# Mixer kernel, three stages on one core: x in falling rows, first sums in one bank, V split where it is read

## The reference

```
w = softmax(weight)                                   # 8 heads x 7 taps
out[b,s,h,:] = sum_k w[h,k] * x[b, s-6+k, h, :]        # stage 1: causal convolution along s
x = out
u = x + (U,V low rank along s): h = (x^T @ U @ V)^T    # stage 2
x = u + relu(u @ w_ch1) @ w_ch2
mixed = real(fft(fft(x, axis=s), axis=d))              # stage 3
u = x + mixed; un = (u - mean) / sqrt(var + 1e-6)
out = u + relu(un @ w_ch1') @ w_ch2'
```

## Time and profile before

| | |
|---|---|
| median of three runs | 1252.08 us |
| the profiled execution's own time | 1252.0 us |
| its span | 1250.2 us |
| mean granted TensorE clock | 0.994 |
| PE busy | 1218.4 us (97%) |
| DVE busy | 823.3 us (66%) |
| ACT busy | 645.3 us (52%) |
| POOL busy | 424.6 us (34%) |
| first `up_slot` of block 0 begins | 42.79 us |

### The profile page before, as it was taken

How to read it: one execution, slowest core, us unless ns; L and a number is a source line. 1 busy time by engine, 2 the same in 40 slices (tenths; PEclk the granted TensorE clock), 3 DMA queues, 4 the chain that set the end, 5 groups by cost and what they waited for, 6 DMA issues and landing times.

```text
span 1250.2 us, 23671 instructions
## 1 busy us (share of the span) xinstructions
PE 1218.4 (97%) x8448; PEld 1193.5 (95%) x8448; DVE 823.3 (66%) x2196; ACT 645.3 (52%) x1603; POOL 424.6 (34%) x542
## 2 busy tenths in 40 slices
PE   6799999999999999999999999999999999999998
PEld 5799999999999999999999999999999999999998
DVE  5555576787766577655557777765666877766654
ACT  5355555444566555445555555544445555554553
POOL 0122352244334245333333244421212344533331
PEclk9799999999999999999999999999999999999999
DMA  8867553244556633224434322222323232232220
GB/s 285 263 207 228 181 161 96 78 151 136 160 161 221 210 112 100 75 69 136 135 96 138 115 92 87 92 69 81 96 87 106 86 101 92 92 94 86 87 68 29
DMA packets 87965, 154.86 MB, mean 124 GB/s; under 512 B 11480, under 2 KB 46915, under 8 KB 87804
## 3 DMA queue, kind: packets, MB, share of 16 engines
q1 hardware_dynamic: 80232, 134.35, 34.3%
q0 software_dynamic: 7616, 18.99, 4.8%
HBM read 94.98 MB, written 63.32 MB: 127 GB/s over the span
## 4 chain that ended last, share of the span: by engine, by line
PE 93%; DVE 2%; DMA 2%; issue 1%; POOL 1%; ACT 1%; SPq 0%; POOLq 0%; ACTq 0%
PE bank L804 20%; PE bank L805 9%; PE bank L785 8%; PE bank L792 7%; PE bank L789 7%; PE bank L793 7%; PE bank L786 7%; PE bank L838 4%; PE bank L808 4%; PE bank L886 3%; PE bank L854 2%; PE bank L909 2%; PE bank L856 2%; PE bank L855 2%; PE bank L807 2%; PE bank L870 1%
## 5 line engine op out<-in xcount | busy, mean ns | idle before, releaser
L981 ACT ACTIVATE ht<-bank 128x384 fp32r<-128x384 f32 x528 | 259.0, 490 | 504.3 <-PE bank L793 502.1
L1165 DVE SCALAR_TENSOR_TENSOR ht<-bank,ht 128x384 fp32r<-128x384 f32 x528 | 293.8, 556 | 338.1 <-ACT ht L981 336.8
L804 PE MATMUL bank<-w,ht 128*128 128x384 f32 x1320 | 418.0, 366 | 0.6 <-DVE ub L1173 0.3
L805 PE MATMUL bank<-w,ht 128*128 128x192 f32 x1320 | 330.8, 251 | 0.0
L1409 POOL TENSOR_TENSOR ub<-ub,tmp 128x576 f32<-128x576 f32 x88 | 125.8, 1430 | 463.9 <-DVE ub L1173 313.9
L804 PEld LDWEIGHTS bank<-w,ht 128*128 128x128 f32 x1320 | 248.5, 188 | 3.8 <-issue 3.1
L805 PEld LDWEIGHTS bank<-w,ht 128*128 128x128 f32 x1320 | 252.0, 191 | 0.0
L785 PE MATMUL bank<-uth,w1h 128*128 128x384 f32 x528 | 188.9, 358 | 0.1
L789 PE MATMUL bank<-utl,w1h 128*128 128x384 f32 x528 | 178.9, 339 | 0.3 <-DVE utl L1190 0.2
L792 PE MATMUL bank<-uts,w1s 128*128 128x384 f32 x528 | 178.6, 338 | 0.3
L786 PE MATMUL bank<-uth,w1l 128*128 128x384 f32 x528 | 178.4, 338 | 0.0
(11 more groups left out here) (116 smaller groups left out, 2220.5 us busy)
## 6 DMA issues: line engine op xcount, KB each, us to landing
f1t<-f_copy SPq DMA_DIRECT2D x44, 396.0 KB, 3.3
ub<-x_two SPq DMA_DIRECT2D x44, 288.0 KB, 3.0
mix<-mixed SPq DMA_DIRECT2D x44, 288.0 KB, 3.3
out<-ub SPq DMA_DIRECT2D x44, 288.0 KB
xin<-in_x SPq DMA_DIRECT2D x12, 864.0 KB, 7.2
x_conv<-xin SPq DMA_DIRECT2D x12, 756.0 KB
vch<-v_split SPq DMA_DIRECT2D x44, 192.0 KB, 2.8
mixed<-rowk SPq DMA_DIRECT2D x88, 74.2 KB
```

The lines of the kernel that those rows point to most:

```text
L804: e.matmul(dn[t][:, 0:2 * D], hh, w2[ph][:, m, :], start=(m == 0), stop=False)
L805: mm = e.matmul(dn[t][:, 0:D], hl, w2[ph][:, m, 0:D], start=False, stop=False)
L981: e.activation(hth[q % 4], up[q % 3][:, 0:TOK], ACT.Relu).then_inc(act_h, 1)
L1165: e.scalar_tensor_tensor(htl[q % 4], up[q % 3][:, 0:TOK], 0.0, hth[q % 4].bitcast(F32), ALU.max, ALU.subtract).then_inc(dve_l, 1)
```

## The change

It has three parts, and some moves that go with them.

1. **Falling rows.** The host lays x out so that a tile's rows fall along the partitions. The band then needs diagonals of the other slant, which the DMA from `taps` gives directly: it writes `band`, and `steep`, DVE's copy and the semaphore `band_set` are gone. The convolved rows come out in the same order as before.
2. **First sums in one bank.** For batch 0 the four pieces of x^T U accumulate in one PSUM bank, from the first matmul of piece 0 to the last of piece 3. DVE's four additions to `tacc` and the three that follow become three on 32x192 elements (`first_sum_t`), at the end. Whoever reuses a buffer of a piece waits for a new semaphore, `pe_t0`.
3. **V's first six tiles.** The portions are now tiles 0 to 5, 6 to 14, 15 to 23 and 24 to 32. Portion 0 is made directly in the two `vch` buffers, and `load_v(0)` and `load_v(1)` are gone. It is still written to DRAM (the other batches read it from there), in block 0, slot 0. It is made after all four pieces, no longer in the third. Portion 1 is made in slots 1 and 2 of block 0, and `store_v(1)` moves to slot 3. `load_v(2)` reads tiles 6 to 8, which now belong to portion 1, and so it waits for both stores.

```
-V_PARTS = [(0, 9), (9, 17), (17, 25), (25, N2)]
+V_PARTS = [(0, 2 * TB), (2 * TB, 15), (15, 24), (24, N2)]
...
-    return x[:, first[None, :] + np.arange(N1)[:, None]]
+    return x[:, first[None, :] + np.arange(N1)[::-1, None]]
...
-        vpart = [ht[0:4 * R, 0:V_PARTS[0][1] * 128], vmid[:], vlate[:], vlate[:]]
+        vpart = [vch[:].rearrange("r k t p -> r (k t p)"), vmid[:], vlate[:], vlate[:]]
...  (SP)
-            e.dma_start(steep[:], bass.AP(taps.tensor, 0, [[1, 128], [QW, H], [1, CT]])).then_inc(steep_in, 16)
+            e.dma_start(band[:], bass.AP(taps.tensor, 0, [[1, 128], [QW, H], [1, CT]])).then_inc(band_in, 16)
...
+                if k == 2:
+                    e.wait_ge(v_stored[0], 16)
...
             store_x(0, 2)
-            store_v(0)
             store_x(0, 3)
             load_w2(0, w2a)
-            e.wait_ge(v_stored[0], 16)
-            load_v(0)
             load_u(0)
-            load_v(1)
             load_u(1)
...
+                    if (n, m) == (0, 0):
+                        store_v(0)
+                    if (n, m) == (0, 3):
+                        store_v(1)
                     if (n, m) == (0, 5):
                         load_v(2)
-                        store_v(1)
...  (PE)
-                e.wait_ge(v_in[k % 2], (k // 2 + 1) * 16)
+                if k < 2:
+                    e.wait_ge(v_l, 1)
+                else:
+                    e.wait_ge(v_in[k % 2], k // 2 * 16)
...
-                o, q = empty(e, ("t", c, p))
+                if c == 0:
+                    q, first, last = 0, p == 0, p == NP - 1
+                    o = tb[q]
+                else:
+                    o, q = empty(e, ("t", c, p))
+                    first, last = True, True
                 for j in range(w):
                     mm = e.matmul(..., start=(first and j == 0), stop=(last and j == w - 1))
-                mm.then_inc(pe_tb[q], 1)
+                mm.then_inc(pe_tb[q] if last else pe_t0, 1)
...
-            e.wait_ge(band_set, 1)
+            e.wait_ge(band_in, 16)
...  (ACT)
-                if p == 2:
-                    v_high(0)
+            v_high(0)
...
-            e.wait_ge(v_stored[0], 16)
...
-                    if m == 4 and n < 3:
+                    if (n, m) in ((0, 1), (1, 4), (2, 4)):
                         v_high(n + 1)
...  (DVE)
+            def first_sum_t():
+                o, q = full(e, ("t", 0, NP - 1))
+                e.tensor_copy(tsum[:, 0, :], o[0:R, 0:D]).then_inc(dve_ts, 1)
+                e.wait_ge(dve_ts, 1)
+                e.tensor_tensor(tsum[:, 1, :], o[0:R, D:2 * D], tsum[:, 0, :], ALU.add).then_inc(dve_ts, 1)
+                e.wait_ge(dve_ts, 2)
+                e.tensor_tensor(tsb[:], o[R:2 * R, 0:D], tsum[:, 1, :], ALU.add).then_inc(tb_free[q], 1)
...
-            e.wait_ge(steep_in, 16)
-            e.tensor_copy(band[:], steep[:, :, ::-1]).then_inc(band_set, 1)
...
-                if p:
-                    sum_t(0, p - 1)
-                if p == 2:
-                    v_low(0)
+            v_low(0)
             weights_low(0)
-            sum_t(0, NP - 1)
+            first_sum_t()
             t_low(0)
...
-                    if m == 4 and n < 3:
+                    if (n, m) in ((0, 2), (1, 4), (2, 4)):
                         v_low(n + 1)
```

More of the change, by code:

```diff
@@ L216, in program @@
         ht = sb("ht", [128, 8 * TOK], F32R)
-        with nc.sbuf_tensor("steep", [128, H, CT], F32) as steep:
-            pass
         qb = sb("qb", [GR, 2, CF], F32)
@@ L383, in fill_both @@
             fill((kind, n, 1), 1, act)
-        for p in range(NP):
-            fill(("t", 0, p), p % 2, False)
+        fill(("t", 0, NP - 1), 0, False)
         fill_both("low", 0, False)
@@ L407, in program @@
         (ld_cw, ld_u, ld_id, ld_back, dve_tl, dve_xf, ld_mir, ld_tab, ld_tabs, cw_ready, eps_set, taps_zero, taps_set,
-         taps_out, steep_in, band_set, u_h, u_l, v_h, v_l, w0_h, w0_l, w1_h, w1_l, cwc,
-         act_un, dve_nm, act_tst, dve_tst, pe_cv, act_x, act_xh, dve_xh, dve_xl, pool_xl, dve_ts,
+         taps_out, band_in, u_h, u_l, v_h, v_l, w0_h, w0_l, w1_h, w1_l, cwc,
+         act_un, dve_nm, act_tst, dve_tst, pe_cv, pe_t0, act_x, act_xh, dve_xh, dve_xl, pool_xl, dve_ts,
          pe_up, act_h, dve_l, pe_dn, pe_dnt, act_p2, dve_y, pool_y,
@@ L413, in program @@
             "ld_cw ld_u ld_id ld_back dve_tl dve_xf ld_mir ld_tab ld_tabs cw_ready eps_set taps_zero taps_set "
-            "taps_out steep_in band_set u_h u_l v_h v_l w0_h w0_l w1_h w1_l cwc "
-            "act_un dve_nm act_tst dve_tst pe_cv act_x act_xh dve_xh dve_xl pool_xl dve_ts "
+            "taps_out band_in u_h u_l v_h v_l w0_h w0_l w1_h w1_l cwc "
+            "act_un dve_nm act_tst dve_tst pe_cv pe_t0 act_x act_xh dve_xh dve_xl pool_xl dve_ts "
             "pe_up act_h dve_l pe_dn pe_dnt act_p2 dve_y pool_y "
@@ L867, in part_of_t @@
                     src = xhl
-                o, q = empty(e, ("t", c, p))
+                if c == 0:
[4 more added lines that the diff above has]
+                    first, last = True, True
                 for j in range(w):
                     mm = e.matmul(o[0:2 * R, 0:2 * D], uhl[0:CT, j0 + j, :], src[0:CT, j].rearrange("p a d -> p (a d)"),
-                                  start=(j == 0), stop=(j == w - 1))
-                mm.then_inc(pe_tb[q], 1)
+                                  start=(first and j == 0), stop=(last and j == w - 1))
+                mm.then_inc(pe_tb[q] if last else pe_t0, 1)
             def convolve(c, p, k):
@@ L1055, in first_high @@
             def first_high(p, k):
-                if p >= 2:
-                    full(e, ("t", 0, p - 2))
+                wait(e, pe_t0, p - 1)
                 e.wait_ge(act_x, pair_of(0, p, k) + 1)
@@ L1077, in t_high @@
             def t_high(c):
-                e.wait_ge(dve_ts, (c + 1) * 3)
-                if c:
+                if c == 0:
+                    taken(e, ("t", 0, NP - 1))
+                else:
+                    e.wait_ge(dve_ts, c * 3 + 2)
                     full(e, ("low", at[(0, c - 1, NB - 1)], 1))
@@ L1287, in sum_t @@
                 if p == 0:
-                    wait(e, dve_ts, c * 3)
+                    e.wait_ge(dve_ts, c * 3 - 1)
                     e.tensor_copy(tacc[:], part).then_inc(tb_free[q], 1)
@@ L1298, in sum_t @@
                         e.tensor_tensor(tsum[:, n, :], half[:, 0:D], half[:, D:2 * D], ALU.add).then_inc(dve_ts, 1)
-                    e.wait_ge(dve_ts, c * 3 + 2)
+                    e.wait_ge(dve_ts, c * 3 + 1)
                     e.tensor_tensor(tsb[:], tsum[:, 0, :], tsum[:, 1, :], ALU.add).then_inc(dve_ts, 1)
@@ L1319, in _ @@
             e.wait_ge(taps_zero, 1)
-            e.tensor_tensor(tap_row[:, :, CT - 1:CT - 1 + K], cw[:], wb(0), ALU.mult).then_inc(taps_set, 1)
+            e.tensor_tensor(tap_row[:, :, N1 - K:N1], cw[:, :, ::-1], wb(0), ALU.mult).then_inc(taps_set, 1)
             def v_low(n):
```

1 line of the change is left out of this document (added).

## The result

| | before | changed |
|---|---|---|
| median of 14 runs | 1250.0 us (1248.76 to 1254.18) | 1253.37 us (1251.44 to 1255.72) |
| ratio | | 1.0023 [1.0013, 1.0032] |
| the profiled execution | 1252.0 us | 1252.18 us |
| first `up_slot` | 42.79 us | 40.81 us |
| start of the low-rank product of block 2 | 59.10 us | 58.34 us |

The changed kernel is slower by 2.8 us between the means (the ratio is that of the means; the medians lie 3.4 apart). That is less than three tenths of a per cent, but 1 lies outside the interval. The forecast was 0.3 us faster. The three runs of before that were shown lie at 1252.08 in the middle; eleven more brought the median to 1250.0. The profiled execution of before, from which the sum was made, was a long one.

What follows compares the result with a forecast made beforehand. PE, busy for 1218.4 of 1250.2 us, was taken as the bound. From 1252.0, minus 3.2 for the head, plus 2.9 for PE's wait for V's tiles 6 to 8, came 1251.7 us, range 1248.5 to 1255.0.

Steps and rivals of the forecast that it cites:

- The band: In the head: DVE's copy goes, PE can begin at 10.2 instead of 10.87, 0.7 us for all that hangs on it.
- The x stores: SP's queue in the head: start 0.95 us earlier, 1.5 us less V ahead; last piece lands at 32.85, not 35.32.
- The operand: `tst` in the head, for PE's low-rank product: ready at 34.9, product ends about 35.9, not the bound at 37.1.
- The first use of V's stored tiles: Block 2's low-rank product: PE waits for tiles 6 to 8, which hands back the head's gain.
- DVE's subtraction: Block 0, V's portion 1: DVE's subtraction at about 50.7, with SP's store right behind it.
- The head: Start of the kernel until block 0's rows land: 40.24 becomes 37.1, a gain of 3.2 us, between 1.0 and 4.3.
- The load of block 0's rows: End of the head: 4.84 us less 0.6 for `vch`'s 192 KB, landing at 37.1; other bound 35.9.
- The hole: PE's wait before block 2's low-rank product: tiles wanted at 59.10 land at 62.0, costing 2.9 us (1.0 to 3.9).
- the copy does stand in front: Queue before the load of tiles 6 to 8: a table copy of 6.1 us delays it; landing taken as 62.0.
- the second way: Landing of tiles 6 to 8 without regard to the table copy, from store and load: 61.1.
- The clock: Behind PE's wait in block 1: forecast assumed no fall to the low level; a fall priced at 2.3 us, chance 0.27.
- the second case: Rival: the clock falls in PE's wait in block 1, slot 0, costing 2.3 us; 1254.0 us, chance 0.27.

Runs made afterwards that it cites:

- copy_behind: The changed kernel with block 2's transform-table copy issued behind the load of V's tiles 6 to 8 instead of ahead; 1251.77 us, 1.0008 of the kernel before.
- v_only: The kernel before with part 3 of the change (V's first six tiles) alone; 1254.95 us, 1.0033 of the kernel before.
- hole_only: The kernel before with the load of V's tiles 6 to 8 put behind the store of V's portion 1; 1254.41 us, 1.0029, and 1256.08, 1.0033.
- rows_first: As `early_tiles`, with block 0's rows loaded ahead of w2 in SP's queue; 1251.04 us, 0.9999 of the kernel before.
- a filled one: PE's wait before block 2's low-rank product filled with unread matmuls: 18 in `hole_only`, 1253.85 us, 1.0023; 12 in the changed kernel, 1252.08, 1.0006.
- the three sets: The changed kernel timed three times against the kernel before: 1253.37 us, 1.0023; 1252.33, 1.0009; 1253.15, 1.0021.
- early_tiles: The changed kernel with V's tiles 6 to 8 also made in the head and stored in block 0 slot 0; 1249.15 us, 0.9987, and 1249.6, 0.9986.
- filling its hole: The changed kernel with 12 unread matmuls ahead of PE's wait before block 2's low-rank product; 1252.08 us, 1.0006 of the kernel before.
- early_load: As `rows_first`, with V's tiles 0 to 8 stored and tiles 6 to 8 loaded early in SP's queue, ahead of table copies; 1248.48 us, 0.9980 of before.

## Why the prediction was wrong

**Right.** The band goes from the path: PE starts at 9.74, forecast 10.2. The x stores: the last piece landed at 32.98, forecast 32.85. The operand stays off the path. The first use of V's stored tiles is what is late next, as a wait of PE for the load of `vch` at about 56 us. DVE's subtraction, forecast at 50.7, was at 50.94. Later blocks are as long as before: from the 4000th matmul of the program to the 8000th it takes 572.2 to 572.3 us in all nine profiles of the two kernels.

**The head**: forecast 3.2, measured 2.7 as a mean. The load of block 0's rows is issued 2.3 us earlier on average (forecast 2.5), and takes 0.3 less (4.9 for 5.2) where 0.6 was taken off for V's 192 KB. It was 2.9 once w2 no longer stood ahead of it, so it was w2 that made this load long, more than the bytes of V in front.

**The hole**: forecast 2.9, measured 2.4 as a mean (2.0 to 2.85). The step "the copy does stand in front" is refuted by `copy_behind`. Store and load alone, 3.5+2.4 (in two profiles 4.4+2.3), were the second way in which the prediction worked it out. It gave 61.1, a hole of 2.0, and it was the right one; the choice between them was wrong. Head and hole were each forecast half a microsecond too large. That the difference between them, 0.3 us, came out as forecast is luck.

**The clock: the step that failed.** The prediction took 1251.7, with the clock at its upper level behind the hole, and gave the fall 0.27. It happened in four of the five profiles of the changed kernel, and behind eight of the ten waits of 2 us and more that any of these kernels had there (the changed kernel four times of five, `copy_behind`, `v_only`, `hole_only` twice; not in `rows_first`). None of the profiles with no wait there, with one of less than 1 us or with a filled one has it. The length alone does not decide: 1.99 us was followed by a fall, 2.03 and 2.39 were not. Its price was 1.5 us and not 2.3. So the second case should have been the forecast. What the prediction held against it, that PE had been full for 12 us before the hole, did not hold the clock. That nothing in the trace of before showed how such a hole ends is not quite so: PE waits 1.62 us there at about 520 us, and one profile of it would have misled, as the last section shows. The rule of the Trainium skill ("TensorE: Matmul & The Clock Gate", "HAM oscillation — how this bites in real kernels"), that a wait for DMA between two bursts can put the array back to its low clock, is borne out by eight of these ten waits. I had weighed it and chosen against it.

**The base.** The sum started from one profiled execution at 1252.0 and three runs with a median of 1252.08. More runs put before at 1250.0 to 1251.2. That is why 1253.37 lies only 1.7 above the forecast and inside the stated range, while the change itself did +1.5 to +3.4 between the medians where -0.3 was forecast. That the number is so near is luck.

**With the measured sizes**: -2.7 for the head and +2.4 for the hole, +1.2 for the clock (1.5 in four of five), are +0.9, where the profiles show +0.75. The timed means of the three sets together give 1.9, the medians of the first set 3.4. Of the 1.9 about 1 us is not explained. The four profiled executions of before average 1251.74, 0.65 above the mean of its timed runs, and the five of the changed kernel 1252.82, 0.1 below theirs; so most of the rest may be that the profiles of before happen to be long ones. Shown is that part 3 makes the loss, that the reordered load alone makes one at least as large, and that without the new dependency the change gains 1.6 to 1.7 us (`early_tiles`). How much of the loss in the changed kernel is the clock's is read from positions only; filling its hole gained nothing in the timed runs.

## What to carry to other kernels

Before a head is shortened or a load is hung behind a new producer, list for each prefetched tile how early it lands: here it was 0.4 us in the first profile, and both edits took from it. A wait of the bounding engine for two or three microseconds costs its length and then, where the clock falls behind it, 1.5 us more here. Where the queue was full, a load's place in it set when it landed, so a new chain is to be issued ahead of the bulk.

## What the hardware did that was not expected

- **One stall lowers the clock in about half of the executions.** Where batch 0 gives way to batch 1, PE waits for DVE in both kernels. The second profile of before, its timeline and a window behind it:

```profile
520.33 0.31 PE L918 MATMUL bank<-tht,bct 99*99 99x196 f32 x1 [1.62 <-DVE ub L1185]
```

```profile
522.00:523.00 1.00, 1.00 (x5) 1.00 (x4) 0.00 (x0) 0.00 (x0) 0.75 (x1) 0.50 0.36 138
```

  The fourth profile of before has the same wait:

```profile
520.52 0.31 PE L918 MATMUL bank<-tht,bct 99*99 99x196 f32 x1 [1.62 <-DVE ub L1185]
```

```profile
522.00:523.00 1.00, 1.00 (x10) 0.99 (x9) 0.15 (x1) 0.19 (x1) 0.55 (x1) 1.00 0.57 217
```

  The same 1.62 us, once followed by the lower level and 5 matmuls in a microsecond, once by the upper and 10. It fell in two of four profiles of before and three of five of the changed kernel. From the 2000th matmul to the 4000th it takes 288.1 and 288.4 us in the profiles of before with the fall, 286.7 and 287.3 in those without. So such a fall can be a part of the scatter of some 4 us between runs, and one profile can't tell whether it belongs to the kernel.
- **A landing takes several times as long in a full queue.** Loads of 192 KB landed 2.3 to 2.6 us after issue once the queue had emptied (the chains above). In the full one of 36 to 56 us loads and stores of that size took 11 to 12 us, and 8.4 us the load that `early_load` issued ahead of the bulk.
